# The up product of the first phase in seven block products for pairs of pieces, in the middle token blocks

## The chip, the cores and the metric

The kernel runs on one core of a Trainium2 chip. The metric is the device time of one execution in microseconds, less being better. The engines are TensorE (PE in the rows; its weight loads are PEld), VectorE (DVE), ScalarE (ACT), GpSimd (POOL) and SyncE (SP), which here only issues transfers.

## The reference

Three stages run one after another, all in float32, on 3072 tokens with 512 features (4 sequences of 768 tokens, 8 heads of 64).

1. A decaying linear attention: `state = gamma*state + k v^T`, `y = scale * q state`, token by token.
2. An expert layer: `h = x @ w_in` (512 to 2048), `g = where(h>=1, h, where(h<=-1, 0, (h+1)^2/4))`, `x = g @ w_out` (2048 to 512).
3. A second layer: `h = x @ w_in` (512 to 1024), `h * softmax(h)`, a layer norm with a gain, and `@ w_out` (1024 to 512).

## The kernel before

The first phase computes stages 1 and 2, the second phase stage 3. Every dense product is done in three passes over numbers that are split into a high part (rounded to the fp32r type) and a low part (what is left): high times high, low weight times high, high weight times low.

In the first phase the tokens are cut into 6 blocks of 512 (BLK): 128 tokens of each of the 4 sequences. FF1 = 2048 is cut into 16 pieces of 128 (FT1). For block `blk` and piece `f`:

- `up` (L383) makes `h` of 128 x 512 in one PSUM bank, `hb[f % 2]`, by 4 (parts of the 512 features) x 3 (passes) = 12 matmuls that are 512 columns wide.
- The gate follows: `clamp` on VectorE (L662), `square` on ScalarE (L506), `larger` on VectorE (L667), `high` on ScalarE (L454), `low` on GpSimd (L734). It uses two buffers, `gate[f % 2]`, so clamp(f) waits until down(f-2) has been done.
- `down` (L413) adds the piece to four accumulators `acc`, 12 matmuls of 512 columns.

TensorE's order is written out by hand: up(f), attention work of slot 2f, down(f-2), attention work of slot 2f+1. While block `blk` goes through its pieces, the attention of block blk+1 is computed in a few of these slots (for its four chunks, one per sequence: scores at slots 6, 12, 18, 24, outputs and state at 8, 14, 20, 26). The result `y` is split into `x` (high and low) by `split_y` at piece 15 on ScalarE and VectorE (L603), behind which the next block's up(0) waits. `evacuate` copies the accumulators out at piece 1 of the next block. Block 0 is special: its first up product is `first_up`, in halves of 256 columns (L400), and the weights are loaded and split in it (`split_weights`, L597 on VectorE, L729 on GpSimd). After block 0 all split weights of stage 2 stay in SBUF.

Every engine works through its own list in order. SyncE does too: a transfer whose wait isn't met holds up the ones behind it. The second phase already uses seven block products for its own up product (L900), with 512 columns; it is not touched.

The last block has 15 such steps; its last piece is done in the second phase.

## Time and profile before

| what | value |
|---|---|
| time, median of 3 runs | 867.35 us (865.98 to 868.62) |
| profiled execution, its time | 866.54 us |
| its span, first to last instruction | 864.7 us |
| TensorE busy | 856.2 us, 99% of the span |
| VectorE, ScalarE, GpSimd busy | 449.8, 332.0, 241.3 us |
| granted TensorE clock, mean | 1.000 |

The profile is of one execution. Matmuls are pipelined, so the length of one in a row (0.39 us for 512 columns) is longer than the distance from one start to the next; a rate is read from starts. Idle time of an engine that others don't wait for costs nothing.

### The profile page before, as it was taken

What the parts mean: (1) busy time and instruction counts of PE and PEld (TensorE: products, weight loads), DVE (VectorE), ACT (ScalarE), POOL (GpSimd) and SP (SyncE); (2) the same over time, 40 slices, a digit from 0 to 9 for tenths busy, and PEclk for the clock granted to TensorE, in tenths of its full rate; (3) what the DMA queues carried; (4) which work ended last, traced back from release to release, by engine and by line L of the source; (5) the groups of instructions that cost most, each with busy time, mean ns of one, the idle gap of its engine ahead of it and who ended that gap; (6) DMA issues with size and microseconds to landing.
All of it is one profiled execution on the core that took longest, in us unless ns stands there. A gap on an engine that the chain in (4) does not pass through costs nothing.

```text
span 864.7 us, 12109 instructions
## 1 busy us (share of the span) xinstructions
PE 856.2 (99%) x4816; PEld 698.6 (81%) x4816; DVE 449.8 (52%) x770; ACT 332.0 (38%) x505; POOL 241.3 (28%) x228
## 2 busy tenths in 40 slices
PE   8999999999999999999999999999999999999998
PEld 7788878888888888888888888888877888888886
DVE  5555443333433333333432334557889899888831
ACT  3333342122311233111321223256476577676542
POOL 2644533223232222322212122227521111221000
PEclk9999999999999999999999999999999999999999
DMA  9921102111111111121021103300055654456451
GB/s 339 376 74 52 49 27 72 49 50 49 49 60 52 49 37 61 49 65 59 0 86 37 37 1 128 116 25 24 27 191 173 178 184 151 147 157 189 129 168 64
DMA packets 50744, 82.85 MB, mean 96 GB/s; under 512 B 5248, under 2 KB 23680, under 8 KB 50688
## 3 DMA queue, kind: packets, MB, share of 16 engines
q1 hardware_dynamic: 50400, 81.82, 28.8%
q8 instruction: 38, 0.62, 0.3%
q10 hardware_dynamic: 288, 0.26, 0.1%
q14 instruction: 18, 0.15, 0.1%
HBM read 56.90 MB, written 25.17 MB: 95 GB/s over the span
## 4 chain that ended last, share of the span: by engine, by line
PE 94%; DVE 3%; issue 1%; ACT 1%; DMA 1%; SPq 0%; POOL 0%; DVEq 0%; ACTq 0%
PE acc L413 30%; PE h L383 30%; PE o_ps L1000 14%; PE p L900 11%; PE att L320 3%; PE att L331 2%; PE att L355 1%; PE att L345 1%; DMA q<-in_q 1%; DVE h L1135 1%; DVE solu L1194 1%; PE acc L331 0%; DVE zT_lo L1226 0%; PE h L400 0%; SPq L219 0%
## 5 line engine op out<-in xcount | busy, mean ns | idle before, releaser
L413 PE MATMUL acc<-g_hi,w 128*128 128x512 f32 x768 | 257.3, 396 | 0.0
L383 PE MATMUL h<-x_hi,w 128*128 128x512 f32 x760 | 249.9, 389 | 0.5 <-DVE x_lo L603 0.5
L734 POOL TENSOR_TENSOR g_lo<-g_raw,g_hi 128x512 fp32r<-128x512 f32 x96 | 126.4, 1316 | 396.1 <-ACT g_hi L454 396.1
L506 ACT ACTIVATE g_raw<-g_raw,half_bias 128x512 f32<-128x512 f32 x96 | 69.5, 724 | 337.1 <-DVE g_raw L662 337.1
L413 PEld LDWEIGHTS acc<-g_hi,w 128*128 128x128 f32 x768 | 144.1, 188 | 35.2 <-issue 3.4
L383 PEld LDWEIGHTS h<-x_hi,w 128*128 128x128 f32 x760 | 142.6, 188 | 30.7 <-DVE x_lo L603 0.9
L662 DVE TENSOR_SCALAR g_raw<-h 128x512 f32<-128x512 f32 x96 | 66.2, 690 | 172.3 <-PE acc L413 172.2
L413 PE MATMUL acc<-g_lo,w 128*128 128x512 f32 x384 | 149.6, 390 | 0.0
L383 PE MATMUL h<-x_lo,w 128*128 128x512 f32 x380 | 147.9, 389 | 0.0
L667 DVE TENSOR_TENSOR g_raw<-h,g_raw 128x512 f32<-128x512 f32 x96 | 66.4, 692 | 69.6 <-ACT g_raw L506 69.6
L454 ACT ACTIVATE g_hi<-g_raw 128x512 fp32r<-128x512 f32 x96 | 60.7, 632 | 72.8 <-DVE g_raw L667 72.8
L413 PEld LDWEIGHTS acc<-g_lo,w 128*128 128x128 f32 x384 | 72.1, 188 | 13.9
L383 PEld LDWEIGHTS h<-x_lo,w 128*128 128x128 f32 x380 | 71.3, 188 | 14.6
L1000 PE MATMUL o_ps<-w_out_hi,zT_hi 128*128 128x512 f32 x192 | 74.9, 390 | 1.7 <-DVE zT_lo L1226 1.7
L1000 PE MATMUL o_ps<-w_out_hi,zT_lo 128*128 128x512 f32 x192 | 74.7, 389 | 0.0
L1000 PE MATMUL o_ps<-w_out_lo,zT_hi 128*128 128x512 f32 x192 | 74.7, 389 | 0.0
L1320 POOL TENSOR_TENSOR rstd<-var,power 128x1 f32<-128x1 f32 x24 | 13.3, 568 | 164.3 <-DVE var L1203 164.3
L1017 ACT ACTIVATE zT_hi<-zt 128x512 fp32r<-128x512 f32 x48 | 27.5, 621 | 43.4 <-DMA zt<-z 43.4
L1000 PEld LDWEIGHTS o_ps<-w_out_hi,zT_hi 128*128 128x128 f32 x192 | 36.0, 188 | 10.0 <-DVE zT_lo L1226 1.7
L1000 PEld LDWEIGHTS o_ps<-w_out_lo,zT_hi 128*128 128x128 f32 x192 | 36.0, 188 | 7.5
L1000 PEld LDWEIGHTS o_ps<-w_out_hi,zT_lo 128*128 128x128 f32 x192 | 36.0, 188 | 7.5
L554 DVE TENSOR_TENSOR pr<-att,mask 128x512 f32<-128x512 f32 x40 | 25.7, 684 | 25.2 <-PE att L320 25.2
(116 smaller groups left out, 1056.2 us busy)
## 6 DMA issues: line engine op xcount, KB each, us to landing
z<-zq SPq DMA_DIRECT2D x24, 512.0 KB, 2.8
zt<-z SPq DMA_DIRECT2D x94, 128.0 KB, 3.1
kT<-in_kT SPq DMA_DIRECT2D x24, 256.0 KB, 2.7
q<-in_q SPq DMA_DIRECT2D x24, 256.0 KB, 2.6
v<-in_v SPq DMA_DIRECT2D x24, 256.0 KB, 2.9
x2T<-y SPq DMA_DIRECT2D x24, 256.0 KB, 2.6
x_raw<-x2T SPq DMA_DIRECT2D x12, 512.0 KB, 5.1
out<-o SPq DMA_DIRECT2D x24, 256.0 KB, 3.8
```

What stands on the lines that cost most here:

```text
L320: last = mm(out[e][:, p * P:(p + 1) * P], kT[half(e), p, :], q[half(e), p, :], start=True, stop=True)
L383: last = mm(hb[f % 2][:, :], ww, xx[:, kt, :], start=kt == 0 and t == 0, stop=kt == KT - 1 and t == 2)
L413: last = mm(acc[m][:, :], ww, gg[:, f % 2, :], start=f == 0 and t == 0, stop=f == FT1 - 1 and t == 2)
L454: return nc.scalar.activation(out, in_, ACT.Copy)
L506: nc.scalar.activation(gate[:, f % 2, :], gate[:, f % 2, :], ACT.Square, bias=half_bias[:, 0:1], scale=0.5).then_inc(sem["squared"], 1)
L554: tt(of("pr", c)[:, e, :, :], by_pair(s_banks(c)[e]), mask[:, e, :, :], ALU.mult)\
L662: nc.vector.tensor_scalar(gate[:, f % 2, :], hb[f % 2][:, :], 1.0, -1.0, ALU.min, ALU.max)\
L667: tt(gate[:, f % 2, :], hb[f % 2][:, :], gate[:, f % 2, :], ALU.max).then_inc(sem["gmax"], 1)
L734: tt(g[1][:, f % 2, :], gate[:, f % 2, :], g[0][:, f % 2, :].bitcast(F32), ALU.subtract)\
L900: last = mm(out[:, :], aa, bb, start=k == 0 and i == 0, stop=k == 1 and i == 2)
L1000: last = mm(op[s % 2][:, :], zz[:, f, :], ww[:, f, :], start=f == 0 and i == 0, stop=f == FT2 - 1 and i == 2)
L1017: return nc.scalar.activation(out, in_, ACT.Copy)
```

## The change

Blocks 1 to 4 (`SEVEN`) no longer call `up` and the old steps but `pair(blk, p)` for p = 0 to 7, which does pieces 2p and 2p+1 together. The 256 x 512 by 512 x 512 product is seen as 2 x 2 blocks of weights (two pieces, two halves of the features) and 2 x 2 blocks of `x` (two halves of the features, 256 left and 256 right tokens: b11, b12, b21, b22), and is made of seven block products in place of eight. Each is 2 x 3 matmuls of 256 columns into half a PSUM bank. VectorE joins them in the SBUF tile `h` (one ScalarE copy and seven additions of 128 x 256), and the gate reads `h` from there instead of PSUM.

The seven products need sums of blocks:

- of the weights: four per pair, S1 to S4, the same for all blocks. They are made in block 0: SyncE loads two pieces once more (`load_pair`, 512 KB), VectorE makes four sums of 128 x 256 (`sums_of_weights`), ScalarE and VectorE split them (`sums_high`, `sums_low`, 128 x 1024 each), and SyncE stores 1 MB (`store_sums`) to a tensor in DRAM. There are eight pairs, at pieces 2, 4, 5, 7, 8, 10, 11, 13, the low part a piece later, in two buffers; the second lies where `x3` is later. In blocks 1 to 4 each pair loads its four sums again (`load_sum`, 4 x 256 KB) into one buffer.
- of `x`: t1 to t4 once for each block, on GpSimd (`sum_of_x`), 128 x 512 each; they and b11, b21, b22 are split by `split_part` in place of `split_y`.

The order of the products and of the preparations:

```diff
+P_ORDER = (1, 2, 6, 7, 5, 3, 4)
+S_FORMS = (2, 3, 1, 4)
+S_USER = (6, 7, 5, 3)
+PREPARE_AT = (2, 4, 5, 7, 8, 10, 11, 13)
...
+X_ORDER = (("t3", "t2", "t4", "b11", "b21", "t1", "b22"), ("b11", "b21", "t3", "t2", "t1", "b22", "t4"))
```

SyncE's new transfers; the loads of the attention's chunks are now placed one by one among them:

```diff
+            def store_sums(i):
+                sp.wait_ge(sem["s_lo"], i + 1)
+                sp.dma_start(s_dram[i].rearrange("n p x -> p n x"),
...
+            def load_sum(q, n):
+                if q:
+                    sp.wait_ge(sem["products1"], made(q - 1, S_USER[n]))
...
+            store_sums(7)
+            for par in range(2):
+                sp.wait_ge(sem["s_stored"][par], 16 * FPAIRS // 2)
+            for n in range(4):
+                load_sum(0, n)
```

TensorE. `have` waits at p = 0 for the low part of a block of `x`, `sums` for a loaded sum of weights; `taken1` counts VectorE's joins, 7 for each pair q, `products1` the products made:

```diff
+            def product(p, weights, block):
...
+                for k in range(2):
+                    for i, (ww, xx) in enumerate(((0, 0), (1, 0), (0, 1))):
+                        last = mm(of_product(p), weights(ww, k), x_part(block, xx)[:, k, :],
+                                  start=k == 0 and i == 0, stop=k == 1 and i == 2)
+                last.then_inc(sem["products1"], 1)
...
+                if q:
+                    pe.wait_ge(sem["taken1"], 7 * q)
+                else:
+                    pe.wait_ge(sem["gmax"], FT1 - 1)
+                have("b11")
+                product(1, block_of(first, 0), "b11")
+                have("b21")
+                product(2, block_of(first, 1), "b21")
+                if q == 0:
+                    pe.wait_ge(sem["gmax"], FT1)
+                have("t2")
+                product(6, sums(0), "t2")
+                have("t3")
+                product(7, sums(1), "t3")
+                attention(blk + 1, 4 * p)
+                down(*divmod(blk * FT1 + 2 * p - 2, FT1))
+                attention(blk + 1, 4 * p + 1)
+                pe.wait_ge(sem["part1"], q + 1)
+                pe.wait_ge(sem["taken1"], 7 * q + 1)
+                have("t1")
+                product(5, sums(2), "t1")
+                have("b22")
+                product(3, sums(3), "b22")
+                pe.wait_ge(sem["taken1"], 7 * q + 3)
+                have("t4")
+                product(4, block_of(second, 1), "t4")
+                attention(blk + 1, 4 * p + 2)
+                down(*divmod(blk * FT1 + 2 * p - 1, FT1))
+                attention(blk + 1, 4 * p + 3)
```

ScalarE's `pair` runs `evacuate` (p = 1), `copy_first` (product 1 into `part`), square and high of the odd piece before, then, at the last pair of blocks 1 to 3 (`more`), the high parts of b11, b21, t3, then square(f), t2, high(f), t1; b22 and t4 follow in the next block's first pair. VectorE's, with f = 2p:

```diff
+                if p == 1:
+                    evacuate(blk - 1)
+                if q:
+                    dve.wait_ge(sem["taken1"], 7 * q)
+                    clamp(*divmod(blk * FT1 + f - 1, FT1))
+                dve.wait_ge(sem["part1"], q + 1)
+                join(q, 2, h[:, 0, LEFT_T], part, 0)
+                join(q, 6, part, part, 1)
+                if q:
+                    larger(*divmod(blk * FT1 + f - 1, FT1))
+                    dve.wait_ge(sem["gmax"], blk * FT1 + f)
+                join(q, 7, part7, part, 2)
+                if p == 0 and blk > 1:
+                    split_part(blk, "b22")
+                    split_part(blk, "t4")
+                attention(blk + 1, 4 * p)
+                attention(blk + 1, 4 * p + 1)
+                if more:
+                    for name in ("b11", "b21", "t3"):
+                        split_part(blk + 1, name)
+                join(q, 5, part, part, 3)
+                join(q, 3, part, part, 4)
+                dve.wait_ge(sem["taken1"], 7 * q + 5)
+                clamp(blk, f)
+                join(q, 4, h[:, 1, LEFT_T], part7, 3)
+                dve.wait_ge(sem["taken1"], 7 * q + 6)
+                tt(part7, of_product(5), part7, ALU.add).then_inc(sem["taken1"], 1)
+                larger(blk, f)
+                if more:
+                    split_part(blk + 1, "t2")
+                    split_part(blk + 1, "t1")
+                if blk == BLOCKS - 2 and p == FPAIRS - 1:
+                    split_y()
+                attention(blk + 1, 4 * p + 2)
+                attention(blk + 1, 4 * p + 3)
```

`join` waits for the product (for product 6: until 7 has been made, for 5: until 3 has) and adds it. In block 0 VectorE and ScalarE run `split_part(1, name)` for the seven names of `X_ORDER[0]` at the start of piece 15, ahead of its clamp and square; `sums_of_weights` and `sums_low` come last in a piece. GpSimd:

```diff
+            def sum_of_x(blk, name):
...
+                pool.wait_ge(sem["y_done"], blk * B)
+                n = 4 * (blk - 1)
+                if blk == 1:
+                    pool.wait_ge(sem["s_stored"][1], 16 * FPAIRS // 2)
+                elif name == "t3":
+                    pool.wait_ge(sem["products1"], made((blk - 1) * FPAIRS - 1, 7))
+                elif name == "t4":
+                    pool.wait_ge(sem["products1"], made((blk - 1) * FPAIRS - 1, 4))
...
             def dense(blk):
+                if blk:
+                    low(blk - 1, FT1 - 1)
                 for f in range(steps(blk)):
+                    if blk == 0 and f == FT1 - 2:
+                        for name in ("t3", "t1", "t2", "t4"):
+                            sum_of_x(1, name)
```

In blocks 1 to 3 GpSimd makes t3 first in pair 7, then low(13), t1, t2, t4, low(14).

## Rows read from the trace of the kernel before

**Rows 1.** The page: busy time by engine, and the chain that ended last.

```profile
PE 856.2 (99%) x4816; PEld 698.6 (81%) x4816; DVE 449.8 (52%) x770; ACT 332.0 (38%) x505; POOL 241.3 (28%) x228
...
PE 94%; DVE 3%; issue 1%; ACT 1%; DMA 1%; SPq 0%; POOL 0%; DVEq 0%; ACTq 0%
```

**Rows 2.** Timeline of TensorE, one dense step: start, length, operation (us).

```profile
313.45 0.39 PE L383 MATMUL h<-x_hi,w 128*128 128x512 f32 x1
...
318.89 0.39 PE L383 MATMUL h<-x_hi,w 128*128 128x512 f32 x1
```

**Rows 3.** Timeline of TensorE, the only 256-wide dense matmuls (first_up).

```profile
16.86 1.12 PE L400 MATMUL h<-x_hi,w 128*128 128x256 f32 x8
17.82 0.64 PE L400 MATMUL h<-x_lo,w 128*128 128x256 f32 x4
18.30 0.40 PE L383 MATMUL h<-x_hi,w 128*128 128x512 f32 x1
```

**Rows 4.** Groups by line and form, whole span: count, busy us, mean ns, idle before.

```profile
L662 DVE TENSOR_SCALAR g_raw<-h 128x512 f32<-128x512 f32 x96 | 66.2, 690 | 172.3 <-PE acc L413 172.2
...
L667 DVE TENSOR_TENSOR g_raw<-h,g_raw 128x512 f32<-128x512 f32 x96 | 66.4, 692 | 69.6 <-ACT g_raw L506 69.6
...
L454 ACT ACTIVATE g_hi<-g_raw 128x512 fp32r<-128x512 f32 x96 | 60.7, 632 | 72.8 <-DVE g_raw L667 72.8
...
L734 POOL TENSOR_TENSOR g_lo<-g_raw,g_hi 128x512 fp32r<-128x512 f32 x96 | 126.4, 1316 | 396.1 <-ACT g_hi L454 396.1
...
L585 DVE TENSOR_TENSOR state<-att,state 128x256 f32<-128x256 f32 x16 | 6.6, 415 | 0.0
...
L1141 DVE TENSOR_TENSOR x_lo<-x_raw,x_hi 128x1024 fp32r<-128x1024 f32 x10 | 12.2, 1218 | 0.5 <-ACT x_hi L1017 0.5
...
L710 POOL TENSOR_TENSOR kn<-kn,tables 128x512 f32<-128x512 f32 x20 | 21.8, 1093 | 1.4 <-DMA kn<-in_kn 1.4
```

**Rows 5.** Timeline of the end of block 0 and the start of block 1.

```profile
109.34 0.39 PE L383 MATMUL h<-x_hi,w 128*128 128x512 f32 x1
...
109.61 0.69 DVE L662 TENSOR_SCALAR g_raw<-h 128x512 f32<-128x512 f32 x1 [3.26 <-PE acc L413]
...
111.10 0.69 DVE L667 TENSOR_TENSOR g_raw<-h,g_raw 128x512 f32<-128x512 f32 x1 [0.79 <-ACT g_raw L506]
...
113.53 3.76 DVE L603 TENSOR_TENSOR x_lo<-y,x_hi 128x512 fp32r<-128x512 f32 x4 [1.74 <-ACT x_hi L454]
...
113.79 1.76 POOL L729 TENSOR_TENSOR w<-w_raw,w 128x512 fp32r<-128x512 f32 x1
...
114.78 0.39 PE L383 MATMUL h<-x_hi,w 128*128 128x512 f32 x1
...
116.14 0.50 PE L383 MATMUL h<-x_hi,w 128*128 128x512 f32 x1 [0.52 <-DVE x_lo L603]
```

**Rows 6.** DMA issues of the page: KB each, median us to landing.

```profile
z<-zq SPq DMA_DIRECT2D x24, 512.0 KB, 2.8
...
kT<-in_kT SPq DMA_DIRECT2D x24, 256.0 KB, 2.7
...
x_raw<-x2T SPq DMA_DIRECT2D x12, 512.0 KB, 5.1
```

**Rows 7.** Windows: us; busy us of PE, PEld, DVE, ACT, POOL; clock; DMA; GB/s.

```profile
15.00:115.00 100.00, 100.00 (x701) 81.17 (x698) 53.55 (x70) 38.74 (x66) 55.40 (x43) 1.00 0.42 145
115.00:222.00 107.00, 106.48 (x661) 86.39 (x660) 39.26 (x59) 26.82 (x42) 29.34 (x27) 1.00 0.15 50
15.00:30.00 15.00, 15.00 (x135) 12.24 (x132) 10.95 (x16) 6.97 (x13) 11.22 (x9) 1.00 1.05 386
```

**Rows 8.** Line L603: ns min/median/max of one, first and last start.

```profile
L603 DVE TENSOR_TENSOR x_lo<-y,x_hi x20: 676/680/1784, 113.5 to 520.9; 128x512 fp32r<-128x512 f32 x20
```

**Rows 9.** Timeline of TensorE's first microseconds (the warm-up matmuls).

```profile
1.19 2.93 PE L434 MATMUL acc<-warm 128*128 128x256 f32 x6 [1.19 <-DVE warm L686]
...
7.66 1.56 PE L434 MATMUL acc<-warm 128*128 128x256 f32 x6
```

More of the change, by code:

```diff
@@ L373, in up @@
             def up(blk, f):
                 n = blk * FT1 + f
-                wait(pe, sem["gmax"], n - 1)
+                if blk and f < 2:
+                    pe.wait_ge(sem["taken1"], 7 * LAST_Q)
+                else:
+                    wait(pe, sem["gmax"], n - 1)
                 if blk == 0:
@@ L444, in _ @@
                 outputs(c)
-            for blk in range(BLOCKS):
-                dense(blk)
+            dense(0)
+            for blk in SEVEN:
+                for p in range(FPAIRS):
+                    pair(blk, p)
+            dense(BLOCKS - 1)
             finish["pe_up"] = lambda: up(BLOCKS - 1, FT1 - 1)
@@ L535, in _ @@
                 split_w_in(f)
-            for blk in range(BLOCKS):
-                dense(blk)
+            dense(0)
+            for blk in SEVEN:
+                for p in range(FPAIRS):
+                    pair(blk, p)
+            dense(BLOCKS - 1)
             finish["act_square"] = lambda: square(BLOCKS - 1, FT1 - 1)
@@ L669, in dense @@
             def dense(blk):
+                if blk:
+                    dve.wait_ge(sem["taken1"], 7 * LAST_Q)
+                    clamp(blk - 1, FT1 - 1)
+                    larger(blk - 1, FT1 - 1)
                 for f in range(steps(blk)):
-                    if f == FT1 - 1 and blk < BLOCKS - 1:
-                        split_y(blk + 1)
+                    if blk == 0 and f == FT1 - 1:
+                        for name in X_ORDER[0]:
+                            split_part(1, name)
@@ L694, in _ @@
                 split_weights(f)
-            for blk in range(BLOCKS):
-                dense(blk)
+            dense(0)
+            for blk in SEVEN:
+                for p in range(FPAIRS):
+                    pair(blk, p)
+            dense(BLOCKS - 1)
             finish["dve_w2_out"] = w2_out_lo
@@ L781, in _ @@
                 scale_kn(c)
-            for blk in range(BLOCKS):
-                dense(blk)
+            dense(0)
+            for blk in SEVEN:
+                for p in range(FPAIRS):
+                    pair(blk, p)
+            dense(BLOCKS - 1)
 def second_phase(nc, block, io, sem, mem, x2_dram, z_dram, finish):
```

275 lines of the change are left out of this document (247 added, 28 removed).

## The prediction

> **What bounds the kernel now.** I read the page's busy times and the chain of waits first: TensorE is busy 99% of the span and is 94% of the chain [rows 1]. So whatever shortens TensorE's stream shortens the kernel, as long as nobody makes TensorE wait; and every wait put on it is paid in full. The windows say the same by stage: in block 1 TensorE is busy for 106.5 of 107 us, at a granted clock of 1.00 (the upper level, 2.4 GHz), VectorE 39.3, ScalarE 26.8, GpSimd 29.3 [rows 7]. Then the timeline gives the two rates that the change trades. A dense step of 24 matmuls of 512 columns takes 318.89 - 313.45 = 5.44 us, 0.2267 each [rows 2]. The kernel has dense matmuls of 256 columns in one place: 12 of them take 18.30 - 16.86 = 1.44 us, 0.120 each [rows 3]. That is more than half of 0.2267 (0.113): each matmul has a fixed part.
>
> **The products: -12.9 us.** A pair of pieces has 24 up matmuls of 512 columns before, 24 x 0.2267 = 5.44 us, and 7 x 2 x 3 = 42 of 256 columns after, 42 x 0.120 = 5.04. That is 0.40 per pair; 4 blocks x 8 pairs = 32 pairs give 12.9. One product in eight is saved, but the narrow form gives back nearly half of it (at 0.113 it would be 22). Down and attention keep their matmuls and places, two units in a pair.
>
> **A pair in the steady state: 0, up to +16.** Time 0 is the start of product 1. Products 1, 2, 6, 7 end at 2.88, down at 5.60, 5 and 3 at 7.04, 4 at 7.76, down at 10.48. Handoffs: 0.27 from TensorE to VectorE (109.34 to 109.61) and some 0.05 between others [rows 5]. A join has the shape of L585, 0.415; clamp and larger are 0.69, high 0.63, low 1.32 [rows 4], and from clamp's end to larger it is 0.80 (square; 110.30 to 111.10). Behind product 3: 7.31, joins 5 and 3 to 8.15, clamp 8.9, join 4 and the seventh addition 9.8 with its waits. The next product 1 waits for that one (`taken1`) and comes at 10.48: 0.6 spare. Larger ends at 10.4, high 11.1, low 12.4; down(f) comes at 13.36: 0.9 spare. For the odd piece: larger 4.3, high 5.0, low 6.3, down at 7.76. So no wait, and VectorE's seven joins of 0.415 (2.9 us a pair) are hidden, since 107 / 8 = 13.4 us of a pair had 39.3 / 8 = 4.9 of VectorE busy [rows 7]. Of the rest, `evacuate` at p = 1 starts as soon as down(15) is done and delays clamp by 1.4 us, within the 1.5 of the odd piece; attention's VectorE work stands behind join 7 or larger, where TensorE does attention too. Sums of weights are issued right behind the product that frees them (2.2 to 7.3) and land in 2.7 us [rows 6], over 5 us early; SyncE's chunk loads and `store_x2` between them wait for slots already passed. If half of the 0.6 spare and more were missing, say 0.5 per pair, that would be 16 us: the upper bound.
>
> On clamp the Trainium skill ("VectorE: DVE Perf Modes", "Why PSUM operands drop a tier") speaks for the change: a float32 operation with one source runs at twice the rate out of SBUF, and clamp now reads `h` there; by its figures I estimate 0.42 us instead of the 0.69 of [rows 4]. No row here shows such a clamp. It would add 0.3 to the spare time of a pair and leave the sum as it is.
>
> **The end of block 0: +12.4 us.** Here is what speaks against the change. GpSimd's four sums of `x` for block 1 wait until the last store of weight sums has landed (`s_stored[1]`, because that buffer lies on `x3`), and product 1 waits for the low parts of t3, t2, t4 and b11, all behind them. Step by step, from [rows 4 to 6]:
> - larger(14) ends at 111.10 + 0.69 = 111.8, as before, since its clamp waits for down(12). Then sums_low(7), 1.22 (128 x 1024, L1141): 113.05.
> - The store of 1 MB in 512 packets. 512 KB land in 2.8 us in one form and 5.1 in another; I take 2.7 (256 KB) plus 0.79 MB at the 386 GB/s of [rows 7], 4.7: 117.8. Ends: 2.8 and 2 x 5.1 = 10.2.
> - Four GpSimd subtractions of 128 x 512 at 1.29 to 1.32 (L734), 5.2: 123.0. Ends: 4 x 1.05 (L710) = 4.2, and 4 x (1.32 + 0.68) = 8.0 if each has to wait for a split of VectorE's.
> - ScalarE's copies of t4 and b11, 2 x 0.62, and VectorE's low part, 0.68: 125.0. Product 1 would start at 114.78, so TensorE idles about 10 us.
> - Product 6 waits for `gmax` of piece 15, whose clamp stands behind all seven split parts on VectorE: b21, t1, b22 (3 x 0.68), clamp 0.69, square 0.80, larger 0.69: 129.3. Without waits it would start at 114.78 + 12 x 0.12 = 116.2. Delay 13.1.
> - Before, block 1 had a stall here too: its fourth matmul starts at 116.14, due at 114.78 + 3 x 0.227 = 115.46 [rows 5]. 0.7 of that goes. Net 12.4.
> With all ends together this is 9.5 to 21. Queued behind the waiting subtractions on GpSimd is low(14), done by about 124.5 and needed only behind product 7 at 130.8; the first loads of sums are issued behind the same store and land before 122.
>
> **Inside block 0: 0, up to +4.** VectorE gets 8 x (4 x 0.415 + 1.22) = 23 us beside 53.6 of 100 [rows 7], ScalarE 8 x 1.05. It fits on average, and clamp(f) has 3 us before up(f+2) asks for it. At pieces 10 to 12 the load of the next two pieces is issued only when the last sums are done and lands 3 to 5 us later, so VectorE runs late by up to 4 us; I count nothing.
>
> **The boundaries inside blocks 1 to 4: +6 (0 to 9).** Before, the split into x was hidden (4 x 0.68 on VectorE within piece 15). Now VectorE has b11, b21, t3 between join 7 and join 5. One such split takes 0.68 us at the median and up to 1.78 [rows 8]; at 113.53 four of them took 3.76 in place of 2.72, with a GpSimd operation beside them that took 1.76 [rows 5], where the like of it takes 1.32 [rows 4]. GpSimd makes its sums just then. Undisturbed they end at 7.5, nothing is late. Disturbed (1.35 each, from high(13) at 5.0 and b11's copy at 5.6) they end at 10.0, the joins' last at 12.3, and product 1 is 1.9 late; then b22 and t4 come 0.8 and 0.3 late for products 3 and 4. 3.0 in all; I take 2.0 for each of three boundaries, nearer to the disturbed end because GpSimd is at work all through that stretch.
>
> **Block 4 to 5: +2.0 (1.5 to 3).** `split_y` now stands behind high(14) on ScalarE: 11.1, first copy 11.7, low part 12.4, against 10.48 when up(5, 0) could start.
>
> **TensorE's clock: +1.4 (0 to 2.7).** Ten idle microseconds occur nowhere in this trace, and the granted clock is 1.00 in every window [rows 7]. But the first six warm-up matmuls take 2.93 us and the same six later 1.56 [rows 9], as at 1.2 instead of 2.4 GHz. I take that difference once, 1.4; the upper end is one down product at half speed, 2.7.
> The Trainium skill says it outright ("TensorE: Matmul & The Clock Gate", "What's actually happening"): an idle TensorE is throttled to half its clock and stays there until it has been busy again for a while. Its own example costs half of the throttled time. With the rule the term is 1.4 or more; if the trace's 1.00 stood, it would be 0.
>
> **Sum.** -12.9 + 12.4 + 0 + 6 + 2.0 + 1.4 = +8.9. The profiled execution had 866.54 us (span 864.7 and 1.8 around it), so 875.4 by the profile; the median of the runs shown is 0.8 above it, so 876.2, say 876.
>
> **The rivals.** 0.3% of 867 is 2.6 us: less than that can't be told from no change.
> - *Forecast, 870 to 884, chance 0.62*: the idle TensorE at the end of block 0 eats the gain, and boundaries add.
> - *The boundaries stay hidden and the first term is at its low end, 0.13*: -12.9 + 9.5 + 0 + 1.5 + 0 = -1.9, so 865 to 869, no change. For it: VectorE has half its time free. Against: [rows 8].
> - *Faster, 0.08*: the end of block 0 is covered. It decides at an idle time of about 7 us there: below it the sum falls under -2.6. At full cover it is -12.9 + 2 = -10.9, 856. That needs the store and the four subtractions in less than 3 us together, while the subtractions alone have rows of 1.05 each; or matmuls of 256 columns at 0.113 (-21.8 instead of -12.9), which [rows 3] speaks against. Either would do.
> - *The joins are the bound, 0.13*: the spare 0.6 in a pair is gone because larger (now with two SBUF sources) runs against low on GpSimd as the splits of [rows 8] do. It decides above 0.6 us lost per pair; at 0.5 beyond that, +16: 892. With half of the pairs so, 884.
> - *The products don't run at 0.12, 0.04*: if each had to wait for its weights (the page counts PEld busy at 81%, 698.6 us over 4816 loads, 0.145 each), 42 x 0.145 = 6.1 a pair, 1.05 more than counted, +34: 910. [rows 3] stands against it with the same type and width.
>
> **Chances and range.** Faster by more than 2.6: 0.08. Within: 0.12. Slower: 0.80. The range 866 to 887 leaves out most of the faster case below and the worst of the joins above. The forecast's own is 870 to 884.
>
> **What would show it.** In the trace after: a gap of 8 to 13 us on TensorE that ends near 125, released by VectorE's split of b11, and another of 2 to 3 before product 6; a start of the four GpSimd subtractions near 118; starts of matmuls of 256 columns 0.120 apart; idle time of 1 to 3 us at each later block's start; steady pairs of 10.5 us without attention, where 10.9 stood. The forecast is wrong if the store lands before 114, if pairs idle inside, or if the granted clock falls for longer than one product.

## The result and the profile after

| kernel | time, median | ratio to before, 95% interval |
|---|---|---|
| before | 867.4 us (865.98 to 868.62) | |
| changed | 902.4 us (901.88 to 903.79) | 1.0406, 1.0386 to 1.0426 |

The change makes the kernel 4% slower. 876.0 was forecast with a range up to 887: the sign was right, the size was not. The profiled execution has a span of 900.1 us (before 864.7), so 35.4 us are to be found where 8.9 were forecast.

The page after, for [rows 1]: busy times, the chain that ended last, and the granted clock in 40 slices of 22.5 us, in tenths.

```profile
PE 855.7 (95%) x5392; PEld 729.3 (81%) x5392; DVE 578.3 (64%) x1046; ACT 355.6 (40%) x557; POOL 270.9 (30%) x244
...
PEclk9999996999999999999999999999999999999999
...
PE 71%; DVE 15%; ACT 5%; issue 4%; SPq 2%; DMA 2%; POOL 1%; ACTq 0%; DVEq 0%; POOLq 0%
```

TensorE is as busy as before (855.7 against 856.2), but the chain is TensorE for 71% of the span in place of 94%: VectorE has 15%. VectorE took on 128.5 us of work. The clock shows a 6 in the slice at 135 to 157 us. All of it points to the stretches where VectorE works for the new products, so the windows come next: first the whole of block 0 (for [rows 7]), then the stretches where TensorE stood still or ran slowly. Columns as in [rows 7].

```profile
15.00:131.00 116.00, 102.94 (x689) 83.83 (x690) 85.78 (x107) 44.52 (x69) 57.43 (x40) 0.96 0.65 224
56.00:64.00 8.00, 3.04 (x16) 2.30 (x16) 7.66 (x9) 1.85 (x3) 4.01 (x3) 0.93 0.11 41
82.00:92.00 10.00, 5.83 (x62) 4.60 (x61) 8.14 (x10) 3.04 (x5) 3.77 (x4) 0.91 0.33 103
107.00:116.00 9.00, 5.07 (x30) 4.16 (x30) 7.92 (x10) 2.52 (x4) 3.95 (x3) 0.90 0.22 79
129.00:144.30 15.30, 2.86 (x13) 2.05 (x11) 6.16 (x6) 4.93 (x9) 8.19 (x6) 0.68 0.39 138
144.30:151.00 6.70, 5.75 (x25) 5.48 (x26) 3.43 (x6) 2.14 (x4) 2.16 (x2) 0.50 0.04 10
250.80:253.70 2.90, 2.90 (x16) 2.90 (x15) 2.02 (x3) 1.52 (x4) 1.22 (x1) 0.50 0.11 7
```

Block 0 is now 116 us where it had 100, with VectorE busy for 85.8 (53.6 before). In three stretches of it TensorE stands still while VectorE is busy for 80 to 96% of the time. After the long gap (131.9 to 144.4) TensorE runs at 0.50, the lower level of 1.2 GHz, and again inside block 2's first pair (250.8 to 253.7).

What VectorE waits for tells how full its list is. The columns are us in all, times, longest; the first two lines are the kernel before in 15 to 115, the next two the changed kernel in 15 to 131:

```profile
DVE g_raw L662 <- PE acc L413: 18.6, 12, 3.3
DVE w L597 <- ACT w L454: 15.8, 13, 1.2
...
DVE g_raw L958 <- PE acc L622: 0.2, 1, 0.2
DVE w L867 <- ACT w L665: 15.8, 13, 1.2
```

Of VectorE's 46.4 idle us in block 0 before, 18.6 were waits for TensorE, ahead of the clamp; 25.7 were waits for ScalarE, ahead of a split of weights (15.8) or of `larger` (9.9), and those come back in the changed kernel (15.8 and 11.0). There 85.8 us of work and 26.8 us of waits for ScalarE fill nearly all of the 116, and VectorE waits for TensorE for 0.2 us in all: it is TensorE that waits for VectorE.

**The steady pair** is the first thing to read without a gap. Timeline of TensorE, the first row of products 1, 2, 6, 7 (24 matmuls), of a down product, of products 5, 3, 4 (18 matmuls), and of the next down:

```profile
236.12 0.40 PE L530 MATMUL h<-x_hi,w 128*128 128x256 f32 x2
...
238.99 0.40 PE L622 MATMUL acc<-g_hi,w 128*128 128x512 f32 x1
...
241.74 0.40 PE L530 MATMUL h<-x_hi,s 128*128 128x256 f32 x2
...
243.86 0.40 PE L622 MATMUL acc<-g_hi,w 128*128 128x512 f32 x1
```

From start to start: 2.87, 2.75 and 2.12 us, and the next down takes 2.75 again. The 42 narrow matmuls are 0.119 apart [rows 3], and the pair takes 10.49 where 10.88 stood. No wait is in it.

**The three gaps inside block 0** look alike. The first, as a timeline of TensorE, VectorE and GpSimd (start, length, operation; in brackets the idle time before it and what ended it):

```profile
51.77 1.16 PE L473 MATMUL att<-q,kT 64*128 64x128 f32 x16
...
56.31 1.37 DVE L867 TENSOR_TENSOR w<-w_raw,w 128x512 fp32r<-128x512 f32 x1 [1.22 <-ACT w L665]
...
57.08 1.75 POOL L1086 TENSOR_TENSOR w<-w_raw,w 128x512 fp32r<-128x512 f32 x1
...
57.60 1.50 DVE L889 TENSOR_TENSOR s_raw<-w_pair 128x256 f32<-128x256 f32 x1
...
58.78 1.22 POOL L1067 TENSOR_TENSOR kn<-kn,tables 128x512 f32<-128x512 f32 x1
59.03 1.26 DVE L890 TENSOR_TENSOR s_raw<-w_pair 128x256 f32<-128x256 f32 x1
60.21 0.41 DVE L892 TENSOR_TENSOR s_raw<-s_raw,w_pair 128x256 f32<-128x256 f32 x1
60.66 0.42 DVE L894 TENSOR_TENSOR s_raw<-w_pair,s_raw 128x256 f32<-128x256 f32 x1
61.00 1.22 DVE L898 TENSOR_TENSOR s_x<-s_raw,s_x 128x1024 fp32r<-128x1024 f32 x1
...
62.13 1.28 DVE L824 TENSOR_TENSOR pr<-att,mask 128x512 f32<-128x512 f32 x2
...
63.56 1.76 PE L484 MATMUL att<-pr,v 128*64 128x128 f32 x14 [4.96 <-DVE pr L824]
```

The scores of chunk 5 were ready at 52.9. Their mask (L824), for which TensorE's next attention stage waits, stands on VectorE behind a weight split, four sums of weights and a low part of the sums, and starts at 62.13. TensorE stood for 4.96 us before L484. And the sums of weights take 1.50 and 1.26 us where GpSimd has an operation at the same time, 0.41 where it has none: they end 0.27 and 0.29 us after GpSimd's operation did (59.10 after 58.83, 60.29 after 60.00).

**The end of block 0**, for [rows 5]: the last low part of the sums, the store's issue, GpSimd's sums of `x`, VectorE's splits, and product 1.

```profile
128.69 1.22 DVE L898 TENSOR_TENSOR s_x<-s_raw,s_x 128x1024 fp32r<-128x1024 f32 x1
...
129.93 0.38 SPq L323 DMA_DIRECT2D w_sums<-s_x  x1
...
134.36 1.26 POOL L1108 TENSOR_TENSOR x_raw<-y 128x512 f32<-128x512 f32 x1 [6.86 <-DMA w_sums<-s_x]
...
138.89 1.27 POOL L1108 TENSOR_TENSOR x_raw<-y,x_raw 128x512 f32<-128x512 f32 x1 [0.17 <-POOL x_raw L1108]
...
140.27 3.34 DVE L874 TENSOR_TENSOR x_lo<-x_raw,x_hi 128x512 fp32r<-128x512 f32 x2 [2.67 <-POOL x_raw L1108]
...
144.36 0.77 PE L530 MATMUL h<-x_hi,w 128*128 128x256 f32 x2 [12.50 <-DVE x_lo L874]
...
148.15 0.80 PE L530 MATMUL h<-x_hi,s 128*128 128x256 f32 x2 [0.90 <-DVE g_raw L963]
```

**A boundary**, here block 1 to 2: GpSimd's sums of `x`, VectorE's splits beside them, the joins behind them, and product 1.

```profile
242.34 3.07 DVE L874 TENSOR_TENSOR x_lo<-y,x_hi 128x512 fp32r<-128x512 f32 x2 [0.76 <-ACT x_hi L665]
...
243.13 1.74 POOL L1108 TENSOR_TENSOR y<-y 128x512 f32<-128x512 f32 x1
...
245.01 1.56 POOL L1108 TENSOR_TENSOR x_raw<-y 128x512 f32<-128x512 f32 x1
...
245.34 1.77 DVE L874 TENSOR_TENSOR x_lo<-x_raw,x_hi 128x512 fp32r<-128x512 f32 x1
...
248.89 0.42 DVE L1003 TENSOR_TENSOR h<-h 128x256 f32<-128x256 f32 x1
...
249.36 0.51 PE L530 MATMUL h<-x_hi,w 128*128 128x256 f32 x2 [2.58 <-DVE h L1003]
```

Three splits take 3.07 + 1.77 = 4.84 us, in place of the 2.04 of three undisturbed ones; the seventh addition (L1003) ends at 249.31, and TensorE has waited for it for 2.58 us. Then the 24 matmuls of products 1, 2, 6, 7 take 4.28 us in place of 2.86, since the clock falls to 0.50 within them.

Where the 35.4 us are, from the starts of TensorE's units in both traces (the first up product starts anywhere from 14.8 to 18.0 us in the kept traces, though no run changes what stands ahead of it, so the first row is a matter of the execution):

| place | measured | forecast |
|---|---|---|
| start of the kernel (first up product) | -0.5 | 0 |
| 32 pairs, 10.49 us each in place of 10.88 | -12.5 | -12.9 |
| inside block 0: gaps of 5.0, 4.2, 4.0, then slow matmuls 1.3, 1.5, 1.4 | +17.4 | 0 |
| end of block 0: gap 12.7, products 3.7, down 0.4, less 0.8 of before | +15.8 | +12.4, clock 1.4 |
| three boundaries, 4.4 each (2.75 gap, 1.4 to 1.6 products, 0.2) | +13.2 | +6 |
| block 4 to 5 | +2.4 | +2.0 |
| rest | -0.4 | |

### The profile page after: what moved, and what is told of

The parts are those of the page before. It is cut to its first block, busy times and chain, and to the rows that moved or that the text cites. A ratio compares the mean times of both kernels' runs of the same rounds, so it can differ in the third digit from the quotient of the medians.

```text
span 900.1 us, 14076 instructions
## 1 busy us (share of the span) xinstructions
PE 855.7 (95%) x5392; PEld 729.3 (81%) x5392; DVE 578.3 (64%) x1046; ACT 355.6 (40%) x557; POOL 270.9 (30%) x244
## 4 chain that ended last, share of the span: by engine, by line
PE 71%; DVE 15%; ACT 5%; issue 4%; SPq 2%; DMA 2%; POOL 1%; ACTq 0%; DVEq 0%; POOLq 0%
PE acc L622 22%; PE h L530 18%; PE o_ps L1399 13%; PE p L1299 10%; PE h L592 3%; DVE x_lo L874 2%; PE att L473 2%; DVE g_raw L963 2%; PE att L484 2%; ACT g_raw L740 1%; DMA w_pair<-in_moe_w_in 1%; DVE s_raw L889 1%; PE att L508 1%; DVE g_raw L958 1%; SPq L298 1%
## 5 line engine op out<-in xcount | busy, mean ns | idle before, releaser
L1091 POOL TENSOR_TENSOR g_lo<-g_raw,g_hi 128x512 fp32r<-128x512 f32 x96 | 129.1, 1344 | 364.4 <-ACT g_hi L665 364.4
L971 DVE TENSOR_TENSOR h<-h 128x256 f32<-128x256 f32 x192 | 81.1, 423 | 130.8 <-PE h L530 92.0
L530 PE MATMUL h<-x_hi,s 128*128 128x256 f32 x512 | 98.1, 290 | 0.9 <-DVE g_raw L963 0.9
L530 PE MATMUL h<-x_hi,w 128*128 128x256 f32 x384 | 73.8, 288 | 20.2 <-DVE x_lo L874 12.5
L530 PEld LDWEIGHTS h<-x_hi,s 128*128 128x128 f32 x512 | 84.8, 198 | 3.6 <-DVE g_raw L963 1.2
L592 PE MATMUL h<-x_hi,w 128*128 128x512 f32 x248 | 81.7, 390 | 2.2 <-DVE x_lo L880 2.2
L622 PEld LDWEIGHTS acc<-g_lo,w 128*128 128x128 f32 x384 | 72.7, 189 | 12.9
L530 PEld LDWEIGHTS h<-x_hi,w 128*128 128x128 f32 x384 | 62.8, 195 | 24.1 <-issue 12.9
L958 DVE TENSOR_SCALAR g_raw<-h 128x512 f32<-128x512 f32 x96 | 49.8, 519 | 46.7 <-PE acc L622 45.4
L530 PE MATMUL h<-x_lo,s 128*128 128x256 f32 x256 | 74.0, 289 | 0.0
L592 PEld LDWEIGHTS h<-x_hi,w 128*128 128x128 f32 x248 | 46.5, 188 | 12.2 <-issue 2.6
L530 PE MATMUL h<-x_lo,w 128*128 128x256 f32 x192 | 55.2, 287 | 0.0
```

The source lines that it names most:

```text
L530: last = mm(of_product(p), weights(ww, k), x_part(block, xx)[:, k, :], start=k == 0 and i == 0, stop=k == 1 and i == 2)
L592: last = mm(hb[f % 2][:, :], ww, xx[:, kt, :], start=kt == 0 and t == 0, stop=kt == KT - 1 and t == 2)
L622: last = mm(acc[m][:, :], ww, gg[:, f % 2, :], start=f == 0 and t == 0, stop=f == FT1 - 1 and t == 2)
L958: nc.vector.tensor_scalar(gate[:, f % 2, :], gelu_in(blk, f), 1.0, -1.0, ALU.min, ALU.max)\
L971: tt(out, of_product(p), other, ALU.add).then_inc(sem["taken1"], 1)
L1091: tt(g[1][:, f % 2, :], gate[:, f % 2, :], g[0][:, f % 2, :].bitcast(F32), ALU.subtract)\
```

## The experiments

The first ten are edits of the changed kernel. Theory A, stated first: inside block 0 TensorE waits because VectorE's list is too long there (the preparation adds work and GpSimd lengthens it), at the end of block 0 it waits for the store, and at the boundaries for VectorE.

**One preparation of eight.**

```diff
-PREPARE_AT = (2, 4, 5, 7, 8, 10, 11, 13)
+PREPARE_AT = (2,)
```

> The changed kernel (902.4 us) with only the first of the eight preparations of weight sums in block 0 (its load, VectorE and ScalarE work and store); all pairs load that one set, so the up products of blocks 1 to 4 are of wrong weights, in the same number, size and order; GpSimd's sums of x for block 1 no longer wait for a store. Theory A: the making of the sums costs the three gaps inside block 0 (5.0, 4.2, 4.0 us and 4.2 us of slow matmuls behind them, 17.4 together) and all of the end of block 0 but the order of the splits, of which about 5 us of the 15.8 stay. Then 875 us (872 to 880), and the three gaps are gone. Rival B: the loads of sums in blocks 1 to 4 (1 MB per pair), not the making, crowd the transfers: these stay, and the time stays over 895.

Measured: 876.1 us, ratio 1.0106 (1.0086 to 1.0126), as Theory A expected (875). The profiled execution was the fastest of four (873.0). Its window of block 0 (columns as above) has no idle TensorE left:

```profile
15.00:112.00 97.00, 97.00 (x684) 78.77 (x683) 53.79 (x72) 37.02 (x61) 55.25 (x42) 1.00 0.49 176
```

At the end of block 0 4.7 + 2.4 us stay, without any store to wait for: the sums and splits of `x` alone are late. With the waits that it brings the preparation costs 26 us.

**The mask first.** Attention's mask stands right behind `larger`, ahead of the sums of weights.

```diff
+                    if blk == 0 and 2 * f + 2 in BASE:
+                        attention(1, 2 * f + 2)
```

> The changed kernel with one edit: in block 0 VectorE masks the scores of slots 6, 12, 18, 24 right behind larger of the piece before, ahead of that piece's split of weights and sums, in place of behind them. No work or transfer is taken away. Theory A: the three gaps inside block 0 come from the order in VectorE's queue alone (TensorE waits for the mask, the mask waits behind 6 us of sums that nobody needs yet): they shrink to under 1.5 us each, the clock stays up, and the time falls by 12 to 16, to 888. Rival C: VectorE has too much work in block 0, in whatever order: the gaps move to the up products (which wait for larger) and the time falls by less than 4, over 898. Rival D: the loads of v and kn are late behind the weight pairs on SyncE: no change.

Measured: 898.0 us, 1.0354 (1.0324 to 1.0384): 4.4 gained, where 14 were at stake. The three gaps before L484 are gone, and ten of 0.6 to 1.5 us (8.1 in all) stand in their place. Three are ahead of up products, as here:

```profile
71.63 0.50 PE L592 MATMUL h<-x_hi,w 128*128 128x512 f32 x1 [0.68 <-DVE g_raw L963]
```

Four are ahead of down products and are put down to GpSimd's split of weights. Each time that split stands behind a low part, which waits for a `high` and so for a `larger` that came late, behind the sums. Two are ahead of scores (0.89 for a load of `kT`, 1.46 for nothing that the profile shows), one ahead of L498. Inside block 0, 11.8 of the 17.4 us stay, though the clock is 1.00 there, and the end of block 0 costs 1.4 more. So the mask was the place where the wait showed, not its cause: seven of the ten new waits go back to a late `larger`. The time fits Theory C of the expectation, at its edge (a fall of 4.4, where it said less than 4), but the waits went to more places than the up products that it named, and up to 2.4 us of them may be SyncE's transfers.

**The other buffer.** The two buffers of the sums are exchanged, so that the sums of `x` wait for the seventh store and not the eighth.

```diff
-                    pool.wait_ge(sem["s_stored"][1], 16 * FPAIRS // 2)
+                    pool.wait_ge(sem["s_stored"][0], 16 * FPAIRS // 2)
```

> The changed kernel with the two buffers of the weight sums exchanged: the last set (7) now lies in the buffer that x3 doesn't share, so GpSimd's sums of x wait for the store of set 6, a piece or two earlier. Theory A: the wait for the last store (6.9 us idle on GpSimd before its first subtraction at 134.4) is what is on the path; it goes, GpSimd starts when it has finished its split of weights at about 127.5, product 1 comes 6 to 7 us earlier and the time falls by 6 to 8, to 895. Rival E: the splits behind the sums and the piece-15 clamp set the end anyway: product 6 moves by less than 2, over 900.

Measured: 894.5 us, 1.0314 (1.0284 to 1.0344), as expected. The wait for the store is worth 8 us: down(13) and the gap behind it take 9.3 us in place of 15.4, so 6.1 of it is the gap, and most of the rest are slow matmuls behind it.

**Joins first at the boundaries.** Only b11 is split ahead of the joins.

```diff
-                    for name in ("b11", "b21", "t3"):
-                        split_part(blk + 1, name)
+                    split_part(blk + 1, "b11")
```

> The changed kernel with VectorE's order changed in the last pair of blocks 1 to 3: behind join 7 only b11 is split, then the joins 5, 3, clamp, join 4 and the seventh addition; b21 comes ahead of larger, then t2, t3, t1 (ScalarE in the same order). Theory F: each boundary loses 2.75 us because product 1 waits for the seventh addition behind three splits (1.35 to 1.8 each beside GpSimd), and 1.6 more because the granted clock falls to 0.50 in the idle time's wake; with the joins first both go for the most part, product 2 and 6 wait up to 1.5 instead, and the time falls by 7 to 10, to 894. Rival G: the same contended splits just move the wait from product 1 to products 2, 6 and 7: the fall is under 3.

Measured: 900.1 us, 1.0379 (1.0348 to 1.0409). Product 1 is in time, but products 6 and 7 wait 1.0 us each, for the low parts of t2 and t3, and the four products take 5.4 us in place of 2.9. A boundary still costs 2.9 us of 4.4, and the time falls by 2.3, under the 3 of Theory G: for the most part the order chooses who is late.

**Small sums of x.** In blocks 2 to 4 GpSimd's sums are replaced by an operation on 8 columns; the splits read other data of the same size, so these blocks' values are not the reference's.

```diff
+                if blk > 1:
+                    few = mem["warm"][:, 0:8]
+                    tt(few, few, few, ALU.subtract).then_inc(sem["x_summed"], 1)
+                    return
```

> The changed kernel with GpSimd's sums of x for blocks 2 to 4 left out (a subtraction of 8 columns of scratch stands in their place, with the same waits); the split parts read a block of y instead, in the same size and order. Everything on VectorE and ScalarE is as in the changed kernel. Theory H: the boundary's 4.3 us come from VectorE's splits waiting for GpSimd (1.35 to 1.77 in place of 0.68); without GpSimd's sums they take 0.68 for the most part, product 1 is less than 0.5 late, and the time falls by 9 to 12, to 892. Rival I: the number of operations ahead of the joins is enough by itself: the gap of 2.65 shrinks by less than 1 and the time stays over 897.

Measured: 894.4 us, 1.0311 (1.0283 to 1.0339), a fall of 8.0 where Theory H expected 9 to 12. A boundary costs 0.5 us in place of 4.4, some 11.6 for three. In the profiled execution 1.3 of it are lost to a later start of the first up product, and 1.6 to slow matmuls behind the wait at block 5, where the clock is 0.59 from 545.2 to 549.0 and the changed kernel had no such fall. Its splits on VectorE in the timeline, for those of 242.34 and 245.34 above:

```profile
243.07 2.58 DVE L874 TENSOR_TENSOR x_lo<-y,x_hi 128x512 fp32r<-128x512 f32 x3 [0.76 <-ACT x_hi L665]
```

Three in 2.58 us, where three took 4.84. The splits and joins there have the same sizes and order as before, so GpSimd's sums are the cause at the boundaries.

**Reordered boundaries, reordered block 0, and both.** Three attempts to mend by order alone.

```diff
-                    sum_of_x(blk + 1, "t4")
...
+                if more:
+                    sum_of_x(blk + 1, "t4")
```

> The changed kernel with other orders at the boundaries of blocks 1 to 5 only: ScalarE copies b11 and b21 ahead of high(13) and all of split_y ahead of square(14); GpSimd runs low(13) ahead of t3, and low(14) ahead of t4; VectorE splits b11, b21 ahead of the joins, t3 (and the first half of split_y) behind the seventh addition, t2 and t1 behind larger, b22 ahead of the next pair's join 2. Theory F: the 4.3 us of each boundary are the order in which contended splits stand before the joins and before larger; now they come in the order TensorE asks for them, while it has 7 us of other work. By the after kernel's durations product 1 is not late, product 6 and 3 by some 0.5 each: 3 x 3.2 + 1.8 = 11 less, 891 (889 to 895). Rival G: contention moves the wait as in the last run: 898 or more.

```diff
-PREPARE_AT = (2, 4, 5, 7, 8, 10, 11, 13)
+PREPARE_AT = (2, 4, 6, 7, 9, 10, 12, 13)
...
+                    if blk == 0 and f in PREPARE_AT:
+                        sums_of_weights(PREPARE_AT.index(f))
```

> The changed kernel with block 0 put in order: preparations at pieces 2, 4, 6, 7, 9, 10, 12, 13, so that the pieces ahead of a mask hold none; the mask right behind larger; sums of weights ahead of the split of weights (which waits for ScalarE anyway); the two buffers exchanged; and at piece 15 b11, b21 first, then clamp, t2, larger, t3, t1, b22, t4. Theory A+C: block 0's loss is VectorE's queue order and its peaks. Of 17.4 us inside block 0 at most 4 stay (VectorE has 74 us of work in 100), of 15.8 at the end at most 4 (product 6 still waits for larger(15) and t2). Then 902.4 - 13.4 - 11.8 = 877 (873 to 883). If VectorE's total work were the limit (rival), more than 8 us of stalls stay inside block 0: 885 or more.

The third has the edits of both:

```diff
+                if more:
+                    sum_of_x(blk + 1, "t4")
...
+PREPARE_AT = (2, 4, 6, 7, 9, 10, 12, 13)
```

> Both of the last two: the changed kernel with the orders of block 0 and of the boundaries mended. If the parts are independent, 902.4 - 25 - 11 = 866 (861 to 874), with the 12.5 us that the products save against some 11 of stalls that stay; it may or may not beat the kernel before. If clock falls made the parts cost more than their gaps, it is nearer to 862.

Measured: 909.6, 897.3 and 902.7 us (ratios 1.0486, 1.0344, 1.0410, intervals within 0.004). All three missed what I expected by 18 us or more, for waits that I had overlooked when I moved steps. In the first, t4's sum went behind GpSimd's last low part, and the low part of t2 may only be written when t4's sum has been made (it reads the same place), so product 6 waited at every boundary:

```profile
257.17 0.80 PE L530 MATMUL h<-x_hi,s 128*128 128x256 f32 x2 [3.85 <-DVE x_lo L875]
```

In the second, SyncE's list held the load of `kT` behind a store of sums that was not yet ready: two gaps of 6.8 and 6.6 us before scores, one of them put down to that transfer. A third, of 7.2 us, stands before product 6 of block 1, which waits for `larger` of piece 15. The group of L473 in block 0:

```profile
L473 PE MATMUL att<-q,kT 64*128 64x128 f32 x62 | 6.3, 358 | 13.4 <-DMA kT<-in_kT 6.8 <-issue 6.6
```

**Block 0 mended alone.** SyncE's transfers in the order in which their waits are met, earlier preparations with their sums ahead of the split of weights, the mask hoisted.

```diff
-PREPARE_AT = (2, 4, 5, 7, 8, 10, 11, 13)
+PREPARE_AT = (2, 4, 5, 6, 7, 9, 10, 12)
```

> The changed kernel with mends (1) and (2) alone, buffers and everything else as in it. The end of block 0, the boundaries and block 5 keep their losses (15.8 - the earlier last store, 13.2, 2.4). Theory J: of the 17.4 us inside block 0 at most 4 stay, and the last store lands some 7 us of piece time earlier, so that the gap at the end shrinks from 12.7 by 5 to 6: 902.4 - 13.4 - 5.5 = 883.5 (880 to 888). Rival K: 892 or more.

Measured: 889.7 us, 1.0264 (1.0243 to 1.0284), between the two theories. 7.7 us stay lost inside block 0; three waits of 2.7, 1.7 and 0.9 are 5.2 of them.

**All sums on VectorE.** The same, with the two buffers exchanged, only b11 split ahead of the joins at the boundaries, and the sums of `x` made by VectorE too, so that GpSimd has only its low parts, its splits of weights and attention beside it.

```diff
+            def sum_of_x(blk, name):
+                dve.wait_ge(sem["y_done"], blk * B)
...
+                tt(x_raw(name), one, other, ALU.subtract).then_inc(sem["x_summed"], 1)
```

> The changed kernel with four mends at once. (1) SyncE's transfers in block 0 in the order in which their waits are met, chunk loads ahead of stores. (2) Preparations at pieces 2, 4, 5, 6, 7, 9, 10, 12 with sums ahead of the split of weights, and the mask behind larger, so that the last set is stored a piece earlier; buffers exchanged. (3) The sums of x on VectorE in place of GpSimd (0.68 us each alone in place of 1.3, and nothing of GpSimd's beside the splits), for block 1 already at piece 13. (4) At the boundaries b11 alone ahead of the joins; split_y as in the run before. What the last runs left: e6's two gaps of 6.8 us stood before scores, whose kT load waited on SyncE behind a store of sums (issued 73.0, landed 79.3); e5's gap of 5.3 us at each boundary stood before product 6, since the split of t2 waits for the sum t4, which had been put behind low(14). Theory J: order and port contention are all of the loss, no bound by total work. Then 4 us stay inside block 0, 2 at its end, 1 at each boundary, 0.5 at block 5: 867.4 - 12.5 + 9.5 - 0.8 = 863.6 (859 to 870). Rival K: VectorE's total work in block 0 (90 us in the 116 us up to 131) is a bound by itself: over 10 us of stalls stay there, 872 or more.

Measured: 879.2 us, 1.0144 (1.0127 to 1.0161): the mends give back 23 of 35 us, but my 863.6 was wrong, and the time is where Theory K put it. Left are 7.9 us inside block 0, 8.8 at its end, 2.1, 2.1 and 3.5 at the boundaries, 0.3 at block 5. The window of block 0, a row of VectorE in it, and the row of TensorE's longest wait there:

```profile
15.00:121.00 106.00, 99.17 (x701) 79.50 (x697) 81.56 (x109) 43.75 (x67) 55.38 (x41) 1.00 0.73 256
...
66.55 0.43 DVE L908 TENSOR_TENSOR s_raw<-w_pair 128x256 f32<-128x256 f32 x1 [3.23 <-DMA w_sums<-s]
...
72.99 0.50 PE L592 MATMUL h<-x_hi,w 128*128 128x512 f32 x1 [2.86 <-DVE g_raw L982]
```

VectorE is busy for 81.6 of 106 us, but Theory K's reason, the total work, is not shown by that. VectorE stands idle for 3.23 us at 66.55 and for 2.97 at 75.91, each time ahead of sums of weights whose buffer still holds the set before the last: the store of that set has not landed. I had put the preparations at pieces 4, 5, 6 and 7 in a row, and there are two buffers. What stands behind the first of these waits is the clamp and the `larger` for which TensorE then waits 2.86 us. The version before has the same two waits (3.57 and 2.85 us), and a gap of 2.68 behind the first. So a part of what stays inside block 0 is a list held up by a transfer, and no run here shows what would be left without it.

**From block 2.** If order can't mend it, the place might. Block 0 is as in the kernel before; block 1 stays in the old form of 512 columns and has the preparation; seven products run in blocks 2 to 4.

```diff
-SEVEN = range(1, BLOCKS - 1)
+SEVEN = range(2, BLOCKS - 1)
...
+PREPARE_AT = (0, 2, 4, 5, 7, 8, 10, 11)
```

> The seven block products start at block 2; block 0 is as in the kernel before, and block 1 is done in the old way with 512 columns while the sums of weights are made in it (at pieces 0, 2, 4, 5, 7, 8, 10, 11). Blocks 2 to 4 are as in the last mended version (sums of x on VectorE). Theory L (the cost is not the preparation itself but its place: in block 0 VectorE was busy 53.6 of 100 us before and 74 to 90 with it, in block 1 it has 39.3 of 107): 24 pairs x 0.39 = -9.4; block 1 without a gap; the start of block 2 0 to 1; boundaries inside 2.1 and 3.5 as measured in e9; block 4 to 5 0.3: -3.0, so 863.5, faster than before (range 861 to 866). Rival M (the preparation makes TensorE wait wherever it stands, through transfers held up behind stores on SyncE, late masks, or GpSimd's low parts beside VectorE's sums): 867 or more, with gaps of 0.7 to 3 us in block 1 before attention's second stages or before up products.

Measured: 866.2 us, 0.9988 (0.9979 to 0.9997). Theory L holds for the place: block 1 has no gap inside with the whole preparation in it (0.52 us at its start, as before). The 866.2 lies just above its range of 861 to 866. Its 863.5 was 2.7 too low, for the start of block 2: product 1 of block 2 waits 1.98 us for b11's low part, which stands behind three other splits, and products 6 and 7 are 0.6 late.

**The start of block 2 mended.** b11 and b21 are split first, and down(14) stands ahead of products 6 and 7.

```diff
+                if q == 0:
+                    down(1, FT1 - 2)
+                    pe.wait_ge(sem["gmax"], 2 * FT1)
                 have("t2")
                 product(6, sums(0), "t2")
```

> The version that starts at block 2, with the start of block 2 mended: the splits of b11 and b21 come ahead of those of t2 and t3, and in the first pair down(14) stands ahead of products 6 and 7. Before this, product 1 of block 2 waited 1.98 us for b11's low part behind three splits on VectorE, and products 6 and 7 took 0.6 us more than 24 matmuls do. Theory L (those waits are only the order of VectorE's list): both go, -2.3 or so, 864 (863 to 865), 0.3% faster than before. Rival N (product 6 waits for larger(15), which can't start its clamp until down(13) is done, or VectorE is late by the five splits so that products 5 or 3 wait instead): a fall of less than 1 us, 865.3 or more.

Measured: 864.7 us (862.76 to 865.82), 0.9963 (0.9950 to 0.9976): faster by 0.4% than before, and by 4% than the changed kernel. Of the 2.8 us lost at the start of block 2, 1.4 stay: the wait of 1.98 is down to 0.16, but product 5 now waits 0.92, which the rival of the expectation had named. The two executions with a mean clock of 1.000 took 862.8, the four with 0.996 to 0.998 took 864.3 to 865.8. The windows of blocks 0 and 1, and a wait of VectorE in block 1:

```profile
15.00:115.00 100.00, 100.00 (x715) 81.36 (x712) 53.63 (x70) 38.60 (x66) 55.27 (x43) 1.00 0.43 150
115.00:222.00 107.00, 106.32 (x666) 86.27 (x665) 74.19 (x104) 36.43 (x53) 33.32 (x27) 1.00 0.51 173
...
DVE g_raw L1004 <- PE acc L632: 15.2, 10, 2.3
```

VectorE has 74.2 us of work in block 1, less than the 85.8 and 81.6 in block 0 of the slow versions. There are no splits of weights beside it, and 15.2 us of waits for TensorE are left ahead of its clamps, where block 0 of the changed kernel had 0.2: TensorE doesn't wait.

## Why the prediction was wrong

**The step that failed is "Inside block 0: 0, up to +4"**, where I counted nothing and 17.4 us were lost. Its argument was an average: 23 us more on VectorE beside 53.6 of 100. Four things were missing in it.
- What the idle time was. The 46.4 idle us were counted as room, but 25.7 of them were waits for ScalarE that come back in every piece; only the 18.6 in which VectorE waited for TensorE were to be had. Even the undisturbed 23 us don't fit in there. The 32 that came do so less: 32.2 + 1.1 (more waits for ScalarE) + 1.6 (for the first load of a pair) - 18.4 (of the 18.6, all but 0.2) = 16.5, close to the 17.4 lost.
- The lengths. I took the undisturbed 0.415 and 1.22. Minimum, median and maximum in ns of the first sum of weights, and of the four low parts in one of the two buffers (the four in the other took 1.22 us each):

```profile
L889 DVE TENSOR_TENSOR s_raw<-w_pair x8: 413/1504/1507, 34.8 to 123.8; 128x256 f32<-128x256 f32 x8
...
L898 DVE TENSOR_TENSOR s<-s_raw,s x4: 2305/2307/2314, 42.5 to 118.9; 128x1024 fp32r<-128x1024 f32 x4
```

  VectorE got 85.8 - 53.6 = 32 us, not 23. [rows 8] showed such lengths, and I had used them for the boundaries only.
- What is queued behind. The preparation comes last in a piece, and the next thing in the list is the mask that TensorE needs. The clamp has 3 us to spare, as I wrote; the mask's deadline I had not worked out. In the first gap its scores were ready at 52.9 and TensorE wanted it at 58.6, so with its own 1.28 us it had 4.3 to spare; VectorE came to it 9.2 us after the scores. "VectorE runs late by up to 4 us" stood in the step, and 4 to 5 us is what each gap has, but that is luck: the step had it from loads that land late, and only one load was waited for, the first, for 1.6 us.
- That it isn't the mask alone: with the mask out of the way only 4.4 us came back, and without seven of the preparations all of it. With the same preparation in block 1, where VectorE had 39 us of work and no weight splits, none of it is lost. That VectorE's list is full in block 0 is shown by these three and by its waits. How much of the loss would go if GpSimd's work beside it were gone was not tried there.

**The other steps.** "The products" was right, -12.5 for -12.9 (the step's own numbers give 12.8), at 0.119 us a matmul. "A pair in the steady state" was right: steady pairs have no waits, so the rival "the joins are the bound" fell.

"The end of block 0" was right in its chain (store, four sums, splits, product 1) and nearly so in size: the store landed in 4.4 us (4.7 forecast), the four sums took 5.8 in all (5.2), the idle time was 12.5 (10 forecast). The difference is behind the sums: the splits of t2 and t4 took 3.34 us, and that of b11 came after them, 4.2 in all, where 2.0 stood. The experiment with one preparation adds that 7 of these 16 us don't come from the store or from a late preparation.

"The boundaries inside blocks 1 to 4" had the right mechanism and was mis-sized: 4.4 each, where 2.0 stood. I had worked out 1.9 for product 1 with splits of 1.35; they took 1.61 on average, 3 x 0.26 more, and TensorE waited 2.58. The 1.1 that I had added for late b22 and t4 did not come (products 5, 3 and 4 take 2.12 us there as elsewhere), so that the waits are near the 3.0 worked out, partly by luck, and 2.0 was taken in its place. The other 1.5 of each is the clock, which the step didn't have. The experiment with small sums shows the mechanism.

"Block 4 to 5" was right, 2.4 for 2.0.

"TensorE's clock" was mis-sized: +1.4 forecast for one place, while slow matmuls cost some 4.2 us inside block 0, about 3 at its end and about 4.5 at the boundaries, 12 in all. I had tied the fall to a gap of 10 us. The windows above show 0.50 after a gap of 2.58 us, and 0.93 to 0.90 over stretches with gaps of 4 to 5. The Trainium skill ("TensorE: Matmul & The Clock Gate", "What's actually happening") says that an idle TensorE drops to half its clock, and the traces agree (0.50). The waits of 2.75 us and more in the changed kernel cost 1.3 to 1.5 times their length: 5.0 + 1.3, 4.0 + 1.4, 2.75 + 1.5.

So of the 26.5 us that were missing, 17.4 are inside block 0, about 7 at the boundaries and 2 at the end of block 0. The range failed for the same reason: its upper end, 887, had only "up to +4" for a place where VectorE's list was known to be late.

The rival "Faster" was added up wrongly as well, without the +6 of the boundaries. By the forecast's own terms full cover gives -12.9 + 6 + 2 = -4.9 and not -10.9, and "Faster" would have needed an end of block 0 of at most 2.3 us, not one with an idle time of about 7.

## What to carry to other kernels

Idle time of an engine is room only where it waits for the engine that bounds the kernel; waits for a third engine in each round stay. So before adding work, add up what the engine waits for, not only how long it is busy (18.6 us here, where 46.4 seemed free). Work that fits has then to be laid out in the in-order list of its engine: for each step behind it that another engine waits for, compare its deadline with the sum of what is ahead, at the lengths that the trace shows beside the other engines' work, not at the undisturbed ones. If an order can't keep all deadlines, move the work to a stage where the engine is idle: here reordering alone came from 1.041 to 1.026 at best, with GpSimd's sums moved to VectorE to 1.014, and the move to block 1 came to 0.999 and, with the start of block 2 mended, to 0.996. And when a step moves in a list, look up who else's data, buffer or queue it now waits for or holds up: my mends met just that in t4's sum, in the load of `kT` and in the stores of the sums.

## What the runs showed of the hardware

- A VectorE operation with two sources in SBUF waits while GpSimd works there: 128 x 256 took 0.41 us alone and 1.50 beside it, and ended 0.27 us after GpSimd's. The Trainium skill ("SBUF — State Buffer", "SBUF: two separate sides") says that one of the two has the shared port for a whole instruction and the other stands still, and these rows agree. GpSimd pays as well: its sum took 1.74 us at a boundary and 1.26 alone.
- The clamp out of SBUF takes 0.43 us at the median in place of 0.69 from PSUM, near the 0.42 that the prediction estimated from the rule of the Trainium skill ("VectorE: DVE Perf Modes", "Why PSUM operands drop a tier"):

```profile
L958 DVE TENSOR_SCALAR g_raw<-h x96: 410/427/693, 18.3 to 648.8; 128x512 f32<-128x512 f32 x96
```

- The clock can fall after much less. In the last version two short gaps stand at the same place of each boundary. At the second one (block 3 to 4) the window of the products that follow has 0.69:

```profile
418.30:422.50 4.20, 2.63 (x19) 2.22 (x18) 4.10 (x6) 1.94 (x4) 1.79 (x1) 1.00 0.00 0
422.50:428.00 5.50, 5.46 (x21) 4.57 (x22) 3.92 (x8) 1.87 (x3) 1.47 (x1) 0.69 0.33 98
...
420.85 0.50 PE L538 MATMUL h<-x_hi,s 128*128 128x256 f32 x2 [0.90 <-DVE x_lo L898]
...
422.55 0.51 PE L538 MATMUL h<-x_hi,s 128*128 128x256 f32 x2 [0.72 <-DVE x_lo L898]
```

  One boundary earlier the same two gaps left the clock at 1.00. What decides between them is open.
